# Sparse attention and two expert layers on one core: sinks inside the key blocks of the first two tiles, own PSUM banks for the opening, masks ahead of inverses, and a share of the normalising on VectorE

## What is computed

```python
# attention: q, k, v are [2, 8, 768, 64]; n_sink = 4, window = 128
scores = scale * np.matmul(q, k.transpose(0, 1, 3, 2))
is_sink = pos[None, :] < int(n_sink)
rel = pos[:, None] - pos[None, :]
in_window = (rel >= 0) & (rel < int(window))
scores = np.where(is_sink | in_window, scores, -1000000000.0)
scores = scores - np.max(scores, axis=-1, keepdims=True)
a = np.exp(scores)
a = a / (np.sum(a, axis=-1, keepdims=True) + 1e-09)
x = np.matmul(a, v)                      # then tokens x 512, 1536 tokens
# first layer: 512 -> 2048 -> 512, leaky ReLU with a slope per hidden channel
h = x @ w_in
x = (np.maximum(h, 0.0) + alpha * np.minimum(h, 0.0)) @ w_out
# second layer: top-1 of 8 experts, capacity 384 tokens, 512 -> 1024 -> 512
y = relu(x[chosen] @ w1[e]) @ w2[e], scaled by the gate, zero where dropped
```

## Time and profile before

| | us |
|---|---|
| median of three runs | 661.55 |
| lowest, highest | 660.63, 662.73 |
| the profiled execution | 661.42 |
| its span in the trace | 659.7 |
| TensorE busy, share of the span | 604.8, 92% |
| VectorE busy | 357.8, 54% |
| ScalarE busy | 285.6, 43% |
| GpSimd busy | 158.5, 24% |

### The profile page before, as it was taken

One profiled execution on the slowest core, in us unless ns is written; L12 is line 12 of the kernel. 1 busy time (PEld: TensorE's weight loads), 2 busy tenths in 40 slices (PEclk: granted clock), 3 DMA queues, 4 the chain that ended last, 5 costly groups with the idle time before them and its releaser, 6 DMA issues.

```text
span 659.7 us, 11745 instructions
## 1 busy us (share of the span) xinstructions
PE 604.8 (92%) x3942; PEld 511.7 (78%) x3942; DVE 357.8 (54%) x1025; ACT 285.6 (43%) x679; POOL 158.5 (24%) x213
## 2 busy tenths in 40 slices
PE   7679899999999999999999999889999879859983
PEld 5568788888888888888888899778787667647772
DVE  4657776565557555655564454545745545463410
ACT  4666454433443334333432211316836556465520
POOL 5662222222222222222221000031112231230112
PEclk9999999999999999999999999989999899879998
DMA  7533430201052302010000400154955866865100
GB/s 209 146 81 106 133 99 17 65 17 34 18 160 65 80 17 65 17 33 17 33 17 1 160 1 0 59 181 146 310 186 181 267 197 196 279 201 191 49 33 18
DMA packets 73393, 67.37 MB, mean 102 GB/s; under 512 B 43012, under 2 KB 49172, under 8 KB 73328
## 3 DMA queue, kind: packets, MB, share of 16 engines
q1 hardware_dynamic: 69488, 57.76, 28.3%
q0 software_dynamic: 3840, 8.77, 4.6%
HBM read 57.75 MB, written 12.58 MB: 107 GB/s over the span
## 4 chain that ended last, share of the span: by engine, by line
PE 81%; ACT 6%; DVE 5%; issue 5%; DMA 1%; ACTq 1%; POOL 0%; DVEq 0%; POOLq 0%
PE bank L807 21%; PE bank L809 20%; PE bank L808 20%; PE bank L797 9%; PE bank L843 4%; PE bank L869 3%; ACT fw L636 2%; ACT wh L615 2%; PE bank L936 2%; DVE wl L1096 1%; DMA fw<-y_scratch,mask 1%; DVE rw L1329 1%; DVE rw L1116 1%; PE bank L883 1%; ACT rw L621 1%
## 5 line engine op out<-in xcount | busy, mean ns | idle before, releaser
L807 PE MATMUL bank<-wh,rw 128*128 128x512 f32 x416 | 169.8, 408 | 10.3 <-issue 6.1
L809 PE MATMUL bank<-wh,rw 128*128 128x512 f32 x416 | 165.1, 397 | 0.0
L808 PE MATMUL bank<-wl,rw 128*128 128x512 f32 x416 | 164.9, 396 | 0.0
L1096 DVE TENSOR_TENSOR wl<-fw,wh 128x512 fp32r<-128x512 f32 x160 | 100.4, 687 | 39.1 <-ACT wh L615 37.0
L807 PE MATMUL bank<-rw,wh 128*128 128x256 f32 x384 | 113.4, 295 | 0.0
L809 PE MATMUL bank<-rw,wl 128*128 128x256 f32 x384 | 108.9, 284 | 0.0
L808 PE MATMUL bank<-rw,wh 128*128 128x256 f32 x384 | 108.7, 283 | 0.0
L717 ACT CAST rw<-fw 128x256 fp32r<-128x256 f32 x96 | 39.0, 406 | 145.6 <-DVE fw L1277 145.5
L807 PEld LDWEIGHTS bank<-wh,rw 128*128 128x128 f32 x416 | 79.9, 192 | 27.9 <-issue 12.6
L809 PEld LDWEIGHTS bank<-wh,rw 128*128 128x128 f32 x416 | 79.4, 191 | 17.8
L615 ACT CAST wh<-fw 128x512 fp32r<-128x512 f32 x160 | 88.2, 619 | 5.6 <-DMA fw<-in_moe_w_dram 2.4
(11 more groups left out here) (113 smaller groups left out, 656.8 us busy)
## 6 DMA issues: line engine op xcount, KB each, us to landing
fw<-in_moe_w_dram SPq DMA_DIRECT2D x128, 256.0 KB
fw<-in_moe_w_in_dram SPq DMA_DIRECT2D x16, 256.0 KB, 3.2
fw<-in_moe_w_out_dram SPq DMA_DIRECT2D x16, 256.0 KB, 2.7
o_sb<-in_q_dram SPq DMA_DIRECT2D x12, 256.0 KB, 3.4
o_sb<-in_k_dram SPq DMA_DIRECT2D x12, 256.0 KB, 3.6
y_scratch<-fw SPq DMA_DIRECT2D x12, 256.0 KB, 2.2
out_dram<-v_or_route SPq DMA_DIRECT2D x12, 256.0 KB, 3.6
v_raw<-in_v_dram SPq DMA_DIRECT2D x11, 256.0 KB, 3.2
```

Source lines behind the costliest of these rows:

```text
L807: pe.matmul(dst, ah, bh, start=start, stop=False, skip_group_check=True)
L808: pe.matmul(dst, ah, bl, start=False, stop=False, skip_group_check=True)
L809: return pe.matmul(dst, al, bh, start=False, stop=stop, skip_group_check=True)
L1096: dve.tensor_tensor(wl[:, hf, col:col + PIECE], staged, f32(wh[:, hf, col:col + PIECE]), ALU.subtract).then_inc(weights_low_split, 1)
```

## The change

- Tiles 0 and 1 of each element are scored over 128 and 256 columns (`width`), with the sinks left visible in their key block (mask, `n_sink` columns set to 0). For them there is no p_sink, no sink transpose, no split of it and no sink matmul; the last `values` matmul closes the sum. The split of the sinks' values moves from tile 0's to tile 2's turn.
- For tiles 0 to 2 (OPENING = 3) q and k are transposed into H_BANK[1] and H_BANK[0], the hidden layer's banks, and split in two parts: pair 0, then pairs 1 to 3. VectorE does the second part behind the mask of the tile's first pair. Tile 1's values go to Y_BANK[1] in place of O_BANK. Alpha is transposed into Y_BANK[0].
- `inverse` and `normalise` go from step 2p+1 to step 2p+2, on VectorE behind the next pair's mask.
- For pairs 4 to 11 VectorE multiplies the second head, right behind the inverse; GpSimd the first.
- The staging ring has four slots throughout; the first pieces are split one in two steps up to 10, without the extra one; the wait for 12 pieces and that for alpha go.
- `keep_busy` issues 8 transposes in place of 9, ahead of p_T and not behind it, and none at steps 16 and 22; before step 0 it issues 5 in place of 7.

```diff
-    STG, STG0, FULL0 = 4, 6, 12
+    STG, EARLY = 4, 10
+    OPENING = TPC + 1
...
+        def q_bank(t):
+            return H_BANK[1] if t < OPENING else P_BANK
+        def k_bank(t):
+            return H_BANK[0] if t < OPENING else S_BANK[1]
+        def value_bank(t):
+            return Y_BANK[1] if t == 1 else O_BANK
+        def parts_of(t, part):
+            if t >= OPENING:
+                return slice(0, PPT)
+            return slice(0, 1) if part == 0 else slice(1, PPT)
+        def has_sinks(t):
+            return t % QT >= 2
+        def sinks_to(t):
+            return sum(has_sinks(x) for x in range(t))
+        def width(t):
+            return (P, 2 * P)[t % QT] if t % QT < 2 else KW
+        def by_vector(p):
+            return PPT <= p < PPT * OPENING
...
         def split_by(n):
-            early = min(max((n + 1) // 2, 0) + (n >= 2), FULL0)
+            early = min(max((n + 1) // 2, 0), EARLY)
             late = sum(1 + k % 2 for k in range(OPEN, n + 1))
...
             def step(c, i, n):
-                for p in range(STG0, NP1):
-                    ring = STG0 if p < FULL0 + STG else STG
-                    if split_by(n - 2) <= p - ring < split_by(n - 1):
-                        load_piece(p)
+                for p in range(split_by(n - 2), min(split_by(n - 1), NP1 - STG)):
+                    load_piece(p + STG)
...
-            made(pool.memset(mask[:, 0, P:2 * P], NEG))
-            made(pool.memset(mask[:, 0:2, 0:n_sink], NEG))
+            made(pool.memset(mask[:, 0:2, 0:n_sink], 0.0))
...
             def normalise(p):
...
-                for a in range(2):
-                    x = prob[:, p % 3, a, 0:2 * P]
+                for a in range(2 - by_vector(p)):
+                    x = prob[:, p % 3, a, 0:min(width(t), 2 * P)]
...
-                p = pair_at(n, 1)
+                p = pair_at(n, 2)
                 if p is not None:
                     normalise(p)
...
+            def qk_high(t):
+                for part in range(1 + (t < OPENING)):
+                    q_high(t, part)
+                    k_high(t, part)
...
             def q_T(t):
                 pe.wait_ge(q_loaded, 16 * (t + 1))
-                if t:
+                if t >= OPENING:
                     pe.wait_ge(probT_evacuated, PPT * t - 2)
+                elif t:
+                    pe.wait_ge(qk_low_split[1][0], t)
...
             def values(p):
...
-                    if t:
-                        pe.wait_ge(x_low_split, t)
+                    if t >= 2:
+                        pe.wait_ge(x_low_split, t - (t == 2))
...
                 if p is not None:
                     scores(p, c, i)
+                if n < OPEN and n % 2 == 0 and n != TPC * H:
+                    keep_busy(8, Y_BANK[1] if n < H + 6 else H_BANK[1])
                 p = pair_at(n, 4)
                 if p is not None:
                     p_T(p, c, i)
...
-                if n < OPEN:
-                    keep_busy(9 if n % 2 == 0 else 0)
...
                 dve.reciprocal(rinv[:, hs], rsum1[:, hs]).then_inc(inverse_sum_done, 1)
+                if by_vector(p):
+                    x = prob[:, p % 3, 1, 0:2 * P]
+                    dve.wait_ge(inverse_sum_done, p + 1)
+                    dve.tensor_scalar(x, x, rinv[:, hs.stop - 1:hs.stop], None, ALU.mult).then_inc(normalised_by_vector, 1)
...
                 if t is not None:
-                    q_low(t)
-                    k_low(t)
-                p = pair_at(n, 1)
-                if p is not None:
-                    inverse(p)
+                    q_low(t, 0)
+                    k_low(t, 0)
...
                 p = pair_at(n, 0)
                 if p is not None:
                     mask_max(p)
+                t = tile_at(n, 0)
+                if t is not None and t < OPENING:
+                    q_low(t, 1)
+                    k_low(t, 1)
+                p = pair_at(n, 2)
+                if p is not None:
+                    inverse(p)
...
-                    if m == 0:
-                        dve.wait_ge(weights_low_split, FULL0)
```

More of the change, by code:

```diff
@@ L206, in sparse_attention_then_two_expert_layers @@
         k_transposed = sem("k_transposed")
[L207 to L210, removed]
+        qk_high_split = [[sem(f"{x}{part}_high_split") for x in "qk"] for part in range(2)]
+        qk_low_split = [[sem(f"{x}{part}_low_split") for x in "qk"] for part in range(2)]
         scores_done = sem("scores_done")
@@ L225, in sparse_attention_then_two_expert_layers @@
         x_low_split = sem("x_low_split")
-        stage_loaded = [sem(f"stage{i}_loaded") for i in range(STG0)]
+        stage_loaded = [sem(f"stage{i}_loaded") for i in range(STG)]
         expert_stage_loaded = [sem(f"expert_stage{i}_loaded") for i in range(STG2)]
@@ L279, in sparse_attention_then_two_expert_layers, with vector_heads, pool_heads @@
         H_BANK, Y_BANK, S_BANK, O_BANK, P_BANK = bk[0:2], bk[2:4], bk[4:6], bk[6], bk[7]
+        def q_bank(t):
[16 more added lines that the diff above has]
+            return PPT <= p < PPT * OPENING
+        def vector_heads(p):
+            return sum(by_vector(x) for x in range(p + 1))
+        def pool_heads(p):
+            return 2 * (p + 1) - vector_heads(p)
         def slots_of(t):
@@ L376, in load_piece @@
                 src, _, _, dst, loaded, _ = piece(p)
-                first, ring = (NP1, STG2) if p >= NP1 else (0, STG0 if p < FULL0 + STG else STG)
+                first, ring = (NP1, STG2) if p >= NP1 else (0, STG)
                 if p >= first + ring:
@@ L421, in _ @@
             load_v(0)
-            for p in range(STG0):
+            for p in range(STG):
                 load_piece(p)
@@ L797, in tr, with keep_busy @@
                 return pe.transpose(dst, src, ident[:, :])
-            def keep_busy(k):
+            def keep_busy(k, bank):
                 for _ in range(k):
-                    tr(H_BANK[1][:, 0:P], ident[:, :])
+                    tr(bank[:, 0:P], ident[:, :])
             def three(dst, a, b, start, stop):
@@ L842, in scores @@
                         ds = slice(a * DH, (a + 1) * DH)
-                        m = pe.matmul(S_BANK[a][:, 0:KW], x[ds, :], y[ds, :], start=i == 0, stop=i == 2)
+                        m = pe.matmul(S_BANK[a][:, 0:width(t)], x[ds, :], y[ds, 0:width(t)], start=i == 0, stop=i == 2)
                         if i == 2:
@@ L957, in _ @@
             pe.wait_ge(constants_made, 2)
-            keep_busy(10)
+            keep_busy(10, Y_BANK[1])
             q_T(0)
             k_T(0)
-            keep_busy(7)
+            keep_busy(5, Y_BANK[1])
             def step(c, i, n):
@@ L968, in step @@
                     pe.wait_ge(small_weights_loaded, 32)
-                    pe.transpose(bk[0][:, 0:NF], alpha_row[:, :], ident[0:NF, 0:NF]).then_inc(alpha_transposed, 1)
+                    pe.transpose(Y_BANK[0][:, 0:NF], alpha_row[:, :], ident[0:NF, 0:NF]).then_inc(alpha_transposed, 1)
                 t = tile_at(n, -1)
@@ L974, in step @@
                 t = tile_at(n, H + 3)
-                if t is not None:
+                if t is not None and has_sinks(t):
                     sinks(t)
@@ L1007, in _ @@
             pe.wait_ge(activation_done, NF * NC)
-            keep_busy(3)
+            keep_busy(3, H_BANK[0])
             for t in range(NT - TPC, NT):
@@ L1070, in _ @@
             slot_T(0)
-            keep_busy(10)
+            keep_busy(10, H_BANK[0])
             expert_in(0, (0,))
@@ L1133, in mask_max @@
                         dve.wait_ge(exp_done, 2 * (p - 2) + a + 1)
-                    dve.tensor_tensor_reduce(masked[:, p % 2, a, :], S_BANK[a][:, 0:KW], mask[:, m, :], -SCALE, 3.0e38,
+                    w = width(t)
+                    dve.tensor_tensor_reduce(masked[:, p % 2, a, 0:w], S_BANK[a][:, 0:w], mask[:, m, 0:w], -SCALE, 3.0e38,
                                              ALU.add, ALU.min, nmax[:, h:h + 1]).then_inc(scores_masked, 1)
```

161 lines of the change are left out of this document (89 added, 72 removed).

## The result

The changed kernel takes **658.36 us** (median of 6 runs, 657.28 to 658.96) against 661.74 of the kernel before (6 runs on the same chip, 660.63 to 663.80): ratio **0.9944**, 95% interval 0.9925 to 0.9963. It is faster, by about 3.5 us and not by 6.7. The profiled execution took 657.53 with a span of 655.8, against 661.42 and 659.7.

A forecast was written before the change was run, and what follows sets the result against it. A loop through all engines was taken to bound the opening, TensorE mostly the rest; 5.3 (opening) + 1.7 (tiles 6 and 7) - 0.3 (weight pieces) = 6.7 us off gave 654.8. Own range 652.5 to 657, wide range 651.5 to 658.8.

The forecast's parts named there:

- First scores and pairs 0 to 9: Opening: first scores some 0.6 us earlier, at about 6.8; masks of pairs 0, 3, 5, 9 at 7.35, 14.8, 21.7, 36.6.
- The filler's price in the loop: Opening, pairs 6 to 10: filler between scores and p_T makes the path 3.5 us a pair, 0.9 of it filler.
- rival B: Opening: ScalarE waits for weight piece 5, or filler costs 0.9 in each of pairs 5 to 10; 657.5; chance 0.15.
- the line on the clock: Opening: filler transposes hold TensorE's clock at 1.00, so the sum takes no clock loss.
- rival A: Opening, step 16 without filler: clock falls for some 4 us, 1.5 to 2 us lost, result 656.5; chance 0.2.
- No single wait there exceeds 1.6 us: Argument against a clock fall at step 16, between k_T of tile 2 and scores 9.
- Tiles 6 and 7: Behind the opening: fewer sink matmuls and transposes and narrower scores save 1.7 us, bounds 0.9 to 2.4.
- Weight pieces: Output sums of f=10 and f=12, steps 33 and 35: two fewer pieces split in advance lose 0.3 us, bounds 0 and 4.
- The stall of tile 3's values: TensorE's wait of about 2.2 us before tile 3's values stays, near 72, V load queued behind a piece load.
- C: V stall goes too, TensorE coming later to step 30 than DVE to step 28's end; 3.8 us more, 651; chance 0.06.
- E: Ties at f=10, f=12 and hidden f=12 lost by more than DVE's margin, steps 33 to 35; slower, 665.8; chance 0.05.

The follow-up runs named there:

- experiment 9: Experiment 1's kernel with q, k and all values back in the old banks and q, k split whole: 665.22 us, ratio 1.0038, opening 45.2.
- experiment 6: Experiment 1's kernel with inverse and normalise back one step behind the scores, inverse ahead of the mask: 656.36 us, ratio 0.9904, opening 36.11.
- Experiment 8: Experiment 1's kernel with the eight fillers behind p_T instead of ahead of it: 655.20 us, ratio 0.9909, opening 37.16.
- experiment 2: Changed kernel without the fillers of steps 0 to 20, one run: 660.41 us, opening 40.0.
- experiment 1: Changed kernel with eight fillers at step 16 as well, in Y_BANK[0]: 655.52 us, ratio 0.9885, opening 36.26.
- experiment 3: Changed kernel with tile 3's V load issued ahead of the weight pieces of its step: 655.04 us, ratio 0.9873, opening 40.1.
- experiment 4: Changed kernel with tiles 6 and 7 back at 260 columns with sink matmuls, masks left, so routing differs: 670.01 us.
- experiment 7: Experiment 1's kernel with GpSimd normalising both heads of all pairs, VectorE none: 655.05 us, ratio 0.9907, opening 37.29.
- experiment 5: Changed kernel with fillers at step 16 and the V load ahead of the weight pieces together: 652.36 us, ratio 0.986, opening 36.49.
- experiment 11: Experiment 1's kernel with only tile 1's values back in O_BANK, one run: 662.19 us, opening 42.3.
- experiment 12: Kernel before the change with only tile 1's values and sink values in Y_BANK[1]: 658.75 us, ratio 0.994, opening 38.2.
- experiment 10: Experiment 1's kernel with tiles 0 and 1 back at 260 columns with sink matmuls, one run, only the opening comparable: opening 46.5 us.

## Why the prediction was half right

**Where the number stands.** 658.36 lies inside the wide range of 651.5 to 658.8, 0.4 under its rim, and outside the 652.5 to 657 of the sum itself. Little more than half of the forecast gain came.

**First scores and pairs 0 to 9: right.** 6.55 where 6.8 stood, and no mask of pairs 0 to 9 off by more than 0.52 (pair 7: 29.0 said, 29.52 measured). The multiply of 256 took 0.35 where 0.4 was estimated, the mask 0.28 in place of 0.42. The first scores are a weak point of it: they move by up to 1 us between runs, and experiment 9, with whole splits, has its first mask at 8.09, experiment 6, with the split in two parts, at 8.07. That the split brings them 0.6 forward isn't shown.

**The filler's price in the loop: right sum, wrong reason.** The "3.5 us a pair" counted the filler's 0.9 as a cost, partly covered by the wait for the inverse. Experiment 8 shows that from mask 7 on, where its clock is 1.00 too, it was covered wholly: behind p_T it makes nothing faster. So rival B's condition (0.9 in each pair) did not exist either, and of the loads ScalarE waited for a weight piece once in the opening, 0.2 us.

**The step that failed is the line on the clock, "so I count fillers as holding the clock and the sum takes no loss".** Its first half is right: experiment 2 takes the fillers away and the clock goes to 0.59. But the sum didn't ask what holds the clock in the one step in which the change leaves the filler out, though rival A did. Rival A happened at its place and at its price: 1.5 to 2 said, 1.9 by experiment 1 (and 3.8 in the longer fall of experiment 3). The row on which I had leaned, 3.38 us in 5.00 at full clock, was denser than the 2.96 in 5.60 that came about. "No single wait there exceeds 1.6 us" was offered against the rival; the longest was 1.10 and the clock fell all the same. That argument counted for more than it should have. The Trainium skill ("TensorE: Matmul & The Clock Gate", HAM oscillation) has bursts of matmuls between waits start slow; the fillers of 1.97 at 36.32 agree, and the values behind the 2.26 us of experiment 1 don't, with 1.00.

**Tiles 6 and 7: nearly right.** 1.7 said, 1.5 by the traces and by experiment 4. Of the parts, the sink matmuls (0.95) and the sink transposes (0.1 each) came as said. The width was too dear: six scores of 128 columns hold TensorE for 0.48 where those of 260 take 0.55, and a pair is 0.08 shorter where 0.15 stood.

**Weight pieces: right in size and place, and a wait beside them that wasn't foreseen.** A loss of 0.3 was put at f=10 and f=12. From the scores of step 32 to those of step 36 the changed kernel takes 15.18 us where the kernel before takes 14.84, and the 0.34 falls on the output sums of steps 33 and 35, 0.2 and 0.1. No gap is marked, but the sum of step 33 starts 0.15 us behind the end of VectorE's subtraction of a piece (from the timelines of VectorE and TensorE in the changed kernel), and that of step 35, at 99.74, 0.14 behind the next:
```profile
91.33 0.69 DVE L1152 TENSOR_TENSOR wl<-fw,wh 128x512 fp32r<-128x512 f32 x1
```
```profile
92.17 0.47 PE L858 MATMUL bank<-wh,rw 128*128 128x512 f32 x1
```
What the sum didn't have is the 0.4 lost before the output sum at 57.24, for VectorE's activation split. Experiment 6 shows that the order of the inverse isn't its cause; experiment 7 cuts it to 0.33, so VectorE's multiplies are part of it.

**The stall of tile 3's values: right.** 2.2 us, issued behind a piece load at 73.15, with a fall to 0.56 behind it; experiments 3 and 5 remove it by the queue's order.

**The expert stage: not foreseen, its cause open.** Of the 4.7 us won by the last logits the profiled execution gives back 0.8 by the end. From the last logits to the end of the span it takes 234.7 us before, 235.6 in the changed kernel, 235.6 and 235.5 in experiments 1 and 3, and 232.2 in experiment 5, with the same code there. The spread is as large as what is to be explained. No experiment took that stage apart, but the traces show where part of it lies. Behind the same wait of 2.65 us, 141 us after the last logits, the changed kernel (first row) has a fall and experiment 5 has none:
```profile
561.50:566.50 5.00, 4.93 (x15) 3.95 (x16) 4.50 (x9) 3.68 (x8) 2.08 (x3) 0.66 0.63 194
```
```profile
555.50:560.50 5.00, 5.00 (x22) 4.11 (x23) 4.57 (x8) 3.61 (x7) 2.08 (x2) 1.00 0.75 221
```
The kernel before has 0.70 there. Over the next stretch experiment 5 wins 1.4 us on the changed kernel by it. With the 235.6 us of the others in place of its 232.2, experiment 5's profiled execution would have taken 652.1 (an estimate), which is the median of its runs. Of the 0.8 between the kernel before and the changed one, 0.4 is there by that wait and the rest 22 us later; what brings it isn't shown.

**The sum** comes out as 3.9 (opening) + 1.5 (tiles 6 and 7) - 0.4 (the wait at 57.24) - 0.3 (f=10 and f=12) - 0.8 (expert stage) = 3.9 for 5.3 + 1.7 - 0.3 = 6.7. Of the 2.8 short, 1.4 lie in the opening (1.9 of clock, less 0.1 for the earlier first mask and 0.3 by which the walk from mask 0 on was too long: 36.55 said, 36.26 in experiment 1), 0.4 in the wait behind the opening, 0.2 in tiles 6 and 7, and 0.8 in the expert stage. Of the other rivals, C (the stall gone) and E (ties lost by 1 us and more) did not happen: the stall is there, and no output sum waits over 0.52.

**What carries the gain** I had listed as one of several: the own bank for tile 1's values. Experiments 9, 11 and 12 put it first. The rest of the change isn't idle, though. Beside the bank alone, with an opening of 38.2 (experiment 12), all the rest wins 2.0 us there once the fillers of step 16 are in (36.26), and 0.1 without them (38.14). Against experiment 1, the opening is 10 us longer with sinks in tiles 0 and 1 (46.5 and 36.26), but that is no price of the sinks by themselves: in the old order with the bank they are there at 38.2; the inverse's place gives nothing and VectorE's share 1.0. These prices can't be added: the parts share one loop, and the loss of any of the large ones opens waits of 2 to 3 us, behind which the clock fell each time (0.60 to 0.79 in experiments 9 to 11).

## What to carry to other kernels

When a chain through all engines sets a stage, look for the accumulator bank that two phases share before counting instructions: here it was one bank, worth as much as the whole change. When fillers keep TensorE's clock up, every step in which one is left out needs its own account of how dense the work around it is; a bound on the longest single wait isn't enough. And if a load stands in a queue behind another that waits for a split, move it ahead: 2.2 us for three lines moved.

## What the runs showed of the hardware

- The clock fell to 1.2 GHz (0.50 over 36 to 38 us) behind a stretch with 2.96 us of work in 5.60 and no wait over 1.10.
- It did not always fall behind a wait: 2.2 us before tile 3's values brought 0.60 and 0.56 in the kernel before and the changed one, and 1.00 in experiment 1 after 2.26. In the expert stage 2.65 us brought 0.66 in the changed kernel and 1.00 in experiment 5.
- Transposes of ident do hold the clock: 0.59 to 0.66 without them (experiment 2). The Trainium skill ("TensorE: Matmul & The Clock Gate", Part 4: PE-mode transpose) says that they don't count as a matmul does; by it the fillers here would be useless, and for the float32 transposes of this kernel the measurement decides against it.
- VectorE's multiply of 128x256 by a column took 0.35 us, where GpSimd takes 0.964.
